# Forty unread products in the routing chain of a fused attention, mixture-of-experts and MLP kernel

## What is computed

```python
bits    = (q @ proj > 0), (k @ proj > 0)            # 6 bits: the bucket of a query, of a key
scores  = q @ k.T / 8, kept where both buckets agree
x       = softmax(scores) @ v                       # 16 heads of 768 rows, 64 wide
logits  = x @ w_gate                                # x as 1536 tokens of 512
e       = argmax(logits)                            # one of 8 experts for each token
y       = softmax(logits)[e] * (relu(x @ w1[e]) @ w2[e])
g       = elu(y @ w_in)                             # 2048 wide
out     = g @ w_out
```

## Time and profile before

| | |
|---|---|
| median of 3 runs | 802.46 us (801.5 to 804.58) |
| the profiled execution | 798.53 us, its span 796.8 us |
| mean granted clock of PE in it | 0.987 |
| PE busy | 769.3 us, 97% of the span |
| DVE busy | 422.2 us, 53% |
| ACT busy | 344.0 us, 43% |
| POOL busy | 359.9 us, 45% |

### The profile page before, as it was taken

How to read it: one execution, slowest core, us unless ns; L and a number is a source line. 1 busy time by engine, 2 the same in 40 slices (tenths; PEclk the granted TensorE clock), 3 DMA queues, 4 the chain that set the end, 5 groups by cost and what they waited for, 6 DMA issues and landing times.

```text
span 796.8 us, 14094 instructions
## 1 busy us (share of the span) xinstructions
PE 769.3 (97%) x4165; PEld 664.4 (83%) x4166; DVE 422.2 (53%) x781; ACT 344.0 (43%) x692; POOL 359.9 (45%) x465
## 2 busy tenths in 40 slices
PE   6999999999999769999999999999999999999996
PEld 4899999999999658888888888888888888888885
DVE  5888888898888774221221223234343444443332
ACT  4878787878888622222222222222222322222221
POOL 3434443444345274999999999148000100010001
PEclk9999999999999869999999999999999999999999
DMA  6567574364554567666657766412000100010001
GB/s 173 140 179 193 128 211 125 97 157 108 135 152 126 170 214 235 205 197 198 209 186 222 235 200 186 150 59 88 14 13 14 53 1 0 1 54 0 1 1 53
DMA packets 72903, 97.24 MB, mean 122 GB/s; under 512 B 32864, under 2 KB 35680, under 8 KB 72864
## 3 DMA queue, kind: packets, MB, share of 16 engines
q1 hardware_dynamic: 62160, 76.36, 33.9%
q10 hardware_dynamic: 8544, 13.27, 5.2%
q0 software_dynamic: 2160, 7.09, 2.4%
HBM read 59.57 MB, written 19.44 MB: 99 GB/s over the span
## 4 chain that ended last, share of the span: by engine, by line
PE 89%; DVE 4%; ACT 2%; issue 2%; POOL 1%; DMA 0%; DVEq 0%; POOLq 0%; SPq 0%; ACTq 0%
PE ps_s L750 14%; PE ps_s L752 14%; PE ps_s L751 14%; PE ps_t L659 6%; PE ps_t L849 5%; PE ps_t L847 5%; PE ps_t L848 5%; PE ps_s L650 4%; PE ps_o L692 4%; PE ps_o L693 3%; PE ps_s L651 3%; PE ps_t L781 2%; PE ps_p L613 1%; PE ps_p L598 1%; DVE stats L1159 1%
## 5 line engine op out<-in xcount | busy, mean ns | idle before, releaser
L588 POOL DMA_INDIRECT out_dram<-out_sb,token_of x12 | 11.6, 969 | 226.6 <-ACT out_sb L1050 223.8
L968 ACT ACTIVATE probs<-ps_s,stats 128x768 f32<-128x768 f32 x96 | 95.2, 991 | 39.1 <-POOL stats L476 38.6
L1159 DVE TENSOR_REDUCE stats<-ps_s 128x1 f32<-128x768 f32 x96 | 91.7, 955 | 19.6 <-PE ps_s L651 17.9
L1168 DVE TENSOR_TENSOR pt_lo<-ps_t,pt_hi 128x384 fp32r<-128x384 f32 x192 | 97.3, 549 | 7.2 <-ACT pt_hi L955 5.6
L955 ACT ACTIVATE pt_hi<-ps_t 128x384 fp32r<-128x384 f32 x192 | 83.4, 489 | 2.8 <-PE ps_t L659 2.6
L659 PE MATMUL ps_t<-ident,probs 128*128 128x128 f32 x576 | 81.8, 276 | 1.0 <-DVE pt_lo L1168 1.0
L474 POOL TENSOR_SCALAR stats<-stats 128x1 f32<-128x1 f32 x96 | 21.1, 220 | 132.6 <-DVE stats L1159 132.4
L1059 ACT ACTIVATE elu_e<-elu_e 128x512 f32<-128x512 f32 x48 | 30.3, 632 | 112.0 <-DVE elu_e L1415 112.0
L533 POOL TENSOR_TENSOR w_lo<-stage,w_hi 128x1024 fp32r<-128x1024 f32 x32 | 76.9, 2403 | 0.0
L533 POOL TENSOR_TENSOR w_lo<-late_stage,w_hi 128x1024 fp32r<-128x1024 f32 x32 | 76.5, 2403 | 0.0
L750 PE MATMUL ps_s<-w_hi,gT_hi 128*128 128x512 f32 x192 | 75.6, 394 | 0.1
(11 more groups left out here) (216 smaller groups left out, 1693.1 us busy)
## 6 DMA issues: line engine op xcount, KB each, us to landing
stage<-in_moe_w_dram SPq DMA_DIRECT2D x72, 256.0 KB, 3.3
late_stage<-in_moe_w_dram SPq DMA_DIRECT2D x56, 256.0 KB, 3.4
key_hi_hi<-query_hi_mask SPq DMA_DIRECT2D x30, 192.0 KB, 3.9
x_slots<-x_rows SPq DMA_DIRECT2D x19, 257.0 KB, 5.3
y_dense<-y_sb ACTq DMA_DIRECT2D x19, 256.5 KB, 3.5
xg<-x_slots ACTq DMA_DIRECT2D x16, 257.0 KB, 4.0
raw_qk<-in_q_dram SPq DMA_DIRECT2D x16, 192.0 KB, 3.2
raw_v<-in_v_dram SPq DMA_DIRECT2D x16, 192.0 KB, 2.4
```

The source lines that it names most:

```text
L1159: v_.tensor_reduce(stats[:, 0, c], ps_s[:, 2 * (s % 2):2 * (s % 2) + 2, 0:HW], AX.XY, ALU.max).then_inc(max_found, 1)
L1168: v_.tensor_tensor(pt_lo[gb][where], ps_t[:, half, 0:HW].rearrange("p (t c) -> p t c", c=P), pt_hi[gb][where].bitcast(F32), ALU.subtract). ...
```

## The change

PE gets a helper `unread(count)`: that many products of 128x128 with 128x512, of `w_hi` with itself, into the bank `ps_s[:, 3]`, which nobody reads. `FILL` places forty: 6 ahead of the wait for `chosen`, 11 ahead of the first row search and 2 ahead of its second half, 13 ahead of the second row search and 3 ahead of its second half, 3 between `turn_xg(0)` and the gates, 2 behind the gates. Nothing else in the chain of routing itself is altered.

Around it, POOL issues gather 1 after three scatters in place of four (`GATHER_AT`); gather 2 stays behind eight. PE does `find_rows(2)` after `hidden(0, 1)`, and `find_gates(2)` after `hidden(1, 0)`. The third tile's masks move in memory to `is_slot_late`, and on DVE `mark(2)` goes behind `take_info(0)` and `take_info(1)`, `find(2)` behind `tile(0)`, `take_info(2)` behind `tile(1)`.

```diff
--- before.py
+++ after.py
@@ -47,6 +47,7 @@
     XC, YC = DM + 2, DM + 1
     FIRST_IN = [11, 15, ST]
     DIRECT = 3
+    GATHER_AT = [0, 3, 8]
     TURN_IN = 13
     SCALE = float(D) ** -0.5
     BIG = 2.0 ** 100
@@ -56,6 +57,7 @@
     ABOVE = 2.0 ** -126
     NOT_ABOVE = -ABOVE * (1 + 2.0 ** -23)
     W_START = 7
+    FILL = [6, 11, 2, 13, 3, 3, 2]
     assert D == 64 and QT == 6 and KD == 4 and FC == DM and KC == KD and NH == 2 and BW == 512
     assert NF * P == 4 * FC and NBITS <= 32 and PPB == KD
 
@@ -197,7 +199,9 @@
         y_sb, expert_end = place("y_sb", [P, YC], F32, c)
         assert expert_end <= names["x_rows"][0], (expert_end, names["x_rows"])
 
-        is_slot, o4 = place("is_slot", [P, DIRECT, TT, P], BF16, names["hid"][0])
+        is_slot, o4 = place("is_slot", [P, 2, TT, P], BF16, names["hid"][0])
+        is_slot_late, _ = place("is_slot_late", [P, TT, P], BF16, names["hidT_lo"][0] + KC * P * 4)
+        slot_marks = [is_slot[:, 0], is_slot[:, 1], is_slot_late]
         assert o4 <= expert_end
         late_stage, c = place("late_stage", [P, 2, 2, FC], F32, expert_end)
         assert c <= names["x_rows"][0]
@@ -554,8 +558,8 @@
             pool.wait_ge(tokens_set, 1)
             pool.wait_ge(x_stored, 16 * 3)
             for t in range(TT):
-                if t % (TT // DIRECT) == 0:
-                    k = t // (TT // DIRECT)
+                if t in GATHER_AT:
+                    k = GATHER_AT.index(t)
                     pool.wait_ge(rows_made, k + 1)
                     g.indirect_dma_start(out=x_direct[:, k], out_offset=None, in_=x_tokens,
                                          in_offset=bass.IndirectOffsetOnAxis(ap=rows_of[:, k:k + 1], axis=0)).then_inc(direct_in[k], 16)
@@ -712,6 +716,11 @@
             pairs(pe, body)
 
 
+            def unread(count):
+                for _ in range(count):
+                    mm(ps_s[:, 3], w_hi[:, 0, 0, 0, 0:P], w_hi[:, 0, 0, 0], start=True, stop=True)
+
+            unread(FILL[0])
             pe.wait_ge(rt, RT_CHOSEN)
             flat = chosen[:, :, :].rearrange("p t e -> p (t e)")
             mm(ps_o[:, 0:(TT + 1) * E], before[:], flat, start=True, stop=False)
@@ -723,23 +732,27 @@
             found = [ps_t[:, 0, 0:5], ps_t[:, 1, 0:5], ps_p[:, 0:5]]
             gates = [ps_t[:, 0, 5:8], ps_t[:, 1, 5:8], ps_p[:, 5:8]]
 
-            def find_rows(k):
+            def find_rows(k, fill=0):
                 for t in range(TT):
+                    if t == QT:
+                        unread(fill)
                     if t % QT == 0:
                         pe.wait_ge(slots_marked, k * 2 + t // QT + 1)
-                    last = mm(found[k], is_slot[:, k, t], token_parts[:, t], start=t == 0, stop=t == TT - 1)
+                    last = mm(found[k], slot_marks[k][:, t], token_parts[:, t], start=t == 0, stop=t == TT - 1)
                 last.then_inc(rows_found, 1)
 
             def find_gates(k):
                 pe.wait_ge(rows_made, k + 1)
                 pe.wait_ge(gates_set, 1)
                 for t in range(TT):
-                    last = mm(gates[k], is_slot[:, k, t], gate_parts[:, t], start=t == 0, stop=t == TT - 1)
+                    last = mm(gates[k], slot_marks[k][:, t], gate_parts[:, t], start=t == 0, stop=t == TT - 1)
                 last.then_inc(gates_found, 1)
 
             pe.wait_ge(last_rows, HALF)
-            find_rows(0)
-            find_rows(1)
+            unread(FILL[1])
+            find_rows(0, FILL[2])
+            unread(FILL[3])
+            find_rows(1, FILL[4])
             pe.wait_ge(rt_plan, 1)
 
             def expert(t):
@@ -802,8 +815,8 @@
                 pe.wait_ge(w_ready, e * EC + (W_START - 6))
                 pe.wait_ge(xg_lo, t + 1)
                 hidden(t, odd, 0, slab)
-                if first:
-                    find_rows(2)
+                if isinstance(t, int) and t == 1:
+                    find_gates(2)
                 if not first:
                     turn_hidden(t - 1, 1)
                     for half in range(2):
@@ -812,11 +825,11 @@
                         expert_out(t - 1, half, slab_before)
                 if not last:
                     turn_xg(t + 1)
-                if first:
-                    find_gates(2)
                 turn_hidden(t, 0)
                 pe.wait_ge(w_ready, e * EC + (W_START - 4))
                 hidden(t, odd, 1, slab)
+                if first:
+                    find_rows(2)
                 if isinstance(t, int) and 0 <= t - TURN_IN < BT:
                     turn_y(0, t - TURN_IN, ps_p)
 
@@ -897,8 +910,10 @@
                     outer_last(blk)
 
             turn_xg(0)
+            unread(FILL[5])
             find_gates(0)
             find_gates(1)
+            unread(FILL[6])
             pe.sem_inc(y_made, 1)
             pe.wait_ge(stage_split, EC * 2)
             tile(0, 0, first=True)
@@ -1276,7 +1291,7 @@
 
             def mark(k):
                 for t in range(TT):
-                    last = v_.tensor_scalar(is_slot[:, k, t], slot_of[:], float(k * P), slots[:, t:t + 1], ALU.add, ALU.is_equal)
+                    last = v_.tensor_scalar(slot_marks[k][:, t], slot_of[:], float(k * P), slots[:, t:t + 1], ALU.add, ALU.is_equal)
                     if t % QT == QT - 1:
                         last.then_inc(slots_marked, 1)
 
@@ -1376,17 +1391,17 @@
             step(v_.tensor_copy(gate_parts[:, :, 1], rest))
             v_.tensor_tensor(gate_parts[:, :, 2], rest, gate_parts[:, :, 1], ALU.subtract).then_inc(gates_set, 1)
             move_xg(0, 0)
+            take_info(0)
+            take_info(1)
             mark(2)
             early_low(0)
             early_low(1)
-            take_info(0)
-            take_info(1)
+            tile(0, 0, first=True)
             find(2)
             early_low(2)
             early_low(3)
+            tile(1, 1, second=True, with_early=EC - 4)
             take_info(2)
-            tile(0, 0, first=True)
-            tile(1, 1, second=True, with_early=EC - 4)
             early_low(EC - 2)
             early_low(EC - 1)
             tile(2, 0)
```

## The result

| | before | changed |
|---|---|---|
| median | 801.86 us (800.75 to 806.34, 20 runs) | 805.62 us (804.26 to 808.91, 20 runs) |
| ratio, 95% interval | | 1.0032 [1.0019, 1.0045] |
| the profiled execution | 798.53 us, span 796.8 us | 805.58 us, span 803.9 us |
| mean granted clock of PE | 0.987 | 0.996 |

A forecast was written before the change was run, and what follows sets the result against it. PE, busy without pause from 300 us on, was taken to bound the kernel, so earlier gains reach the end. 1.1 us plus 0.6 for the clock made -1.7: 802.46 to 800.8 us, range 798.6 to 803.2.

The forecast's parts named there:

- The rival in which they are too long: Forty products in the routing chain's gaps overrun at half clock, making searches late: 807.0 us, chance 0.05.
- Without that move PE would wait 1 us here: After the first half tile: unless gather 1 is issued one scatter earlier, PE waits 1 us for its rows.
- The second rival: The clock falls after all, in the thin stretch from 282.5 to 287: 802.3 us, chance 0.20.
- The sum's term for a later return of the clock: Later clock return in typical runs costs only the kernel before: gain between 0 and 1.6 us, taken as 0.6.
- (a): Ahead of the first half tile: shorter transposes and faster draining start it 0.4 us earlier (0 to 0.8), at 287.5.
- (b): First half tile at full clock: 2.86 us in place of 4.64, 1.8 us gained, ending at 290.4.
- (c): From the first half tile's end to `turn_hidden`: 1.0 us in place of 1.10, so it begins at 291.4.
- The four gate sums, 0.8 us: On DVE after the subtraction at 285.9: four sums, some 0.2 us apart, before marks and the L1367 pair.
- The second wait: `turn_hidden(0, 1)` waits for ScalarE's Relu, starting at 298.65: PE ahead by 1.1 us, not 1.7 (bounds 0.7 and 1.7).
- (d): To the next `turn_hidden`: 6.06 us plus 0.6 for moved search and gates; PE free at 298.0, 1.7 us ahead.
- The third gather: Rival: its issue, held by DVE's pair until 297.6, lands late; wait up to 0.8 us, 801.6 us, chance 0.10.
- the sum's 1.1 us: Gain against the profiled execution after PE's wait for Relu near 298.65: 798.53 us falls to 797.4.

The follow-up runs named there:

- the products alone: The kernel before with the forty products and none of the moves: 797.81 us, ratio 0.9923 with late signals; 798.72 us, 0.9982 without.
- the changed kernel without lateness: The changed kernel, unedited, measured again in a set where no signal was late: 798.63 us, ratio 0.9981 to the kernel before.
- Weights first: Changed kernel with DVE's mark(2), early_low(0) and (1) back ahead of take_info(0) and (1): 797.94 and 798.92 us; 798.98 us with late signals.
- the scatters held: Changed kernel with POOL waiting for hid_made before the nine scatters behind the second gather: 798.98 us; 800.23 us, ratio 0.9952, with late signals.

## Why the prediction was wrong

- **The products and their gaps: right.** Eleven took 2.79 us (2.6 forecast), thirteen 3.22 (3.1); the waits for marks fell from 8.5 us to 1.4. The rival in which they are too long fell, and so did "Without that move PE would wait 1 us here": with the products alone, where the second gather isn't moved, the transposes of tile 1 start 0.48 us behind the start of the row search (290.69, 291.17), against 0.32 before.
- **The clock: right until PE ran dry.** 1.00 through the chain. Its fall at 295.75 follows from the wait, it doesn't cause it: PE had had nothing to do since 291.5. The second rival named the wrong place. The sum's term for a later return of the clock (0 to 1.6 us) has rows behind it now: in two more traces of the kernel before the clock returned at 291.16 and 294.22, and the first half tile took 4.34 and 5.29 us, against 291.76 and 4.64.
- **(a) mis-sized.** The first half tile began at 287.87 and 287.98 (the second figure without late signals), not at 287.5, and before at 287.94: the 0.4 us isn't there. 0.58 and 0.39 us of "issue" stand ahead of it, where PE's register load lies. **(b) right**: 2.85 us.
- **(c) failed in the measured set.** "ScalarE's Relu alone fills most of that, so I take 1.0: 291.4." From the end of the half tile to `turn_hidden(0, 0)` it was 5.58 us in the measured set (to 296.30) in place of 1.0. Where signals were on time the step is right: 0.91 us (to 291.75, the 0.35 us above 291.4 being (a)'s).
- **"The four gate sums, 0.8 us": here the forecast failed first.** They were counted as work and not as a wait. Before, they stood behind the marks and the pair of L1367, over 4 us behind their products; afterwards nothing stood between, and DVE waited 5.85 and 2.40 us. No rival had a late signal in it. This is the cover that the section on the change should have named. Where nothing is late the step is right: 286.82 and 289.61, where 289.3 to 289.6 was forecast.
- **Where the 7 us went.** Set against the changed kernel without lateness (span 796.8 us, this one 803.9): 4.55 us from 291.75 to 296.30; the transposes and `hidden(0, 1)` at half clock, 0.76 + 3.82 us in place of 0.41 + 2.85, 1.3 us; from the row search to the second `turn_hidden` 5.85 us in place of 4.69, 1.2 us, as the Relu there stood behind a load that DVE's late pair had released. Together 7.0.
- **The second wait, and term (d): wrong in size even where nothing is late.** `turn_hidden(0, 1)` stood at 299.70, forecast 298.65, and before 299.74: in this pair of traces the 1.1 us isn't there. The load behind the pair landed at 298.10, not near 297, but the wait for the Relu that it made is 0.26 us; PE itself came at 299.44, where (d) had 298.0. The moved search and gates were to cost 0.6 us. From the start of the search to tile 1's first product it is 1.10 us (295.01 to 296.11), with 0.65 us idle in it:

```profile
295.01 0.46 PE L741 MATMUL ps_p<-token_parts,is_slot_late 128*128 128x5 bf16 x12
296.11 0.49 PE L763 MATMUL ps_s<-w_hi,xgT_hi 128*128 x1 [0.65 <-issue]
```

  PE's register load for tile 1 starts at 294.93, and with the search moved only 0.3 us of small products stands between it and the products that need it. Weights first has the same gap in all three sets (0.62, 0.67 and 0.76 us) and no wait for this Relu, and `turn_hidden` stood at 299.29, 299.77 and 299.70. Where the search isn't moved there is no such gap: with the products alone `turn_hidden` stood at 298.50, 1.2 us ahead. With the scatters held in the last set the loads were done earlier, the search took 0.34 us, and PE waited 1.20 us for the Relu that began at 299.38. So in these traces the moved search takes back most of what the products gain, even where nothing is late; this is read from the rows, as no run moved the search alone. The medians of the two (798.63 and 798.72) don't tell the two apart.
- **The third gather: it came without a wait, and the estimate by the rule is not borne out.** Its issue without late signals, and DVE's pair beside it:

```profile
295.64 2.35 DVE L1382 TENSOR_TENSOR w_lo<-late_stage,w_hi 128x1024 fp32r<-128x1024 f32 x2
```
```profile
296.00 1.72 POOL L564 DMA_INDIRECT x_direct<-x_tokens,rows_of  x1 [0.64 <-DVE rows_of L1309]
```

  It took 1.72 us in place of 0.99 and ended at 297.72, before the pair did (297.99), and PE turned its rows at 305.68 without waiting. The prediction had it held until the pair's end, then at 297.6, with its own time still to come. It was through 0.86 us behind the end of the first of the two subtractions (296.86), as if it had got in between them. The issues of 3.10, 2.87 and 2.86 us above were through 0.8 to 0.9 us behind the end of the whole pair, as the one of 2.38 us was. The Trainium skill, SBUF — State Buffer, section "SBUF: two separate sides", says of GpSimd and a DVE instruction with two SBUF inputs that one holds off the other for the whole instruction: the trace agrees for one instruction, but what decides whether two in a row hold an issue off once or twice isn't shown. The kernel before had a row for it too, a scatter beside the pair of 293.22 to 295.57:

```profile
293.99 1.28 POOL L564 DMA_INDIRECT x_slots<-x_rows,pos  x1 [0.30 <-issue]
```

- **"Runs of one kernel differ by more than the sum."** The median shown, 802.46 us, stood 3.9 us above the profiled execution, and this was put down to the clock (0.6) and to scatter. It was the sign that mattered. The trace came from an execution in which nothing was late (798.53; the sets without lateness have 799.3 and 800.1), the median did not. The chain it was read for is the one in which those 3 us were lost. Against a kernel before of 800.09 the change gave -1.5 us, near the -1.7 of the sum; against one of 801.86 it gave +3.8. That the first is near is luck, as far as the rows go: the sum's 1.1 us isn't in the traces, and where the 1.5 us of the medians come from isn't shown.

The version to keep is the forty products without the moves: 0.9923 [0.9898, 0.9947] where signals are late, 0.9982 [0.9973, 0.9991] where they are not. Weights first comes near it (0.9930; 0.9984 and 0.9994).

## What to carry to other kernels

An instruction that waits for another engine belongs behind work that its own engine can do meanwhile, even where the trace shows the signal on time: the place of two lines on DVE decided 8 to 9 us here (by ratios from different sets), and under 1 us where nothing was late. An operation moved for one engine's sake can uncover another's: the moved search left 0.65 us of a register load bare. When the median lies further above the profiled execution than the effect that is forecast, take traces of several executions first, since the trace may show a kernel that the median doesn't. And measure a change beside its baseline more than once: this one was 0.3% slower in one set and 0.2% faster in another, both intervals clear of no change.

## What was not expected of the hardware

- Signals of PE to DVE and ScalarE came up to 9 us behind their products (`gates_found(1)` of the changed kernel: products through by 286.7, signal at 295.42). Signals between 274 and 285.5 were on time, with four indirect transfers issued among them; the lateness began as they went on. In five kernels that kept a row of scatters running to 293.8, 293.8, 294.0, 294.4 and 294.7, `hid_made` came at 295.5, 295.6, 295.7, 296.2 and 296.4: 1.7 to 1.8 us behind the end of the last issue. This is a coincidence in time in five traces; the run with the scatters held is what speaks for a cause.
- It came in the set of the result and in two of four others (kernel before at 801.9, 804.3 and 804.8 us), and not in the rest (799.3 and 800.1). What differs between them isn't known; a late and an undisturbed set ran on the same chip. Their traces have one more mark: some 240 to 310 of 9370 semaphore records are missing, more than half of them between 284 and 304 us. Whether the recording of the trace has a part in the lateness was not tested.
- Open is where PE's signal is held up: on its way, or because the product's last write is late. Matmul ends in a trace are modelled and can't tell this.
- A pause in the row of indirect transfers, made by a wait, lets the signals through: DVE waited 1.26 us in place of 5.85 with the scatters held. With the products alone the pause came from a scatter's issue of 3.10 us beside DVE's pair, and `hid_made` was on time at 290.81.
